# Expert up-products of a fused RWKV and two-stage MoE kernel: order of the first products, their waits, and the place of one row load

## The reference, cut to what matters

```python
for e in range(E):                       # 8 experts
    mask = e_idx == e                    # argmax of x @ w_gate
    h = np.maximum(x[mask] @ w1[e], 0.0) # 384 -> 1024
    ye = h @ w2[e]                       # 1024 -> 384
    out[mask] = gate_w[mask, None] * eom[mask, e, None] * ye
```

## Time and profile before

| | us |
|---|---|
| median of three runs | 867.23 |
| the profiled execution | 865.66 |
| its span, first to last instruction | 863.8 |
| TensorE busy | 842.6 (98%) |
| VectorE busy | 511.0 (59%) |
| ScalarE busy | 320.1 (37%) |

### The profile page before, as it was taken

The page is one execution under the profiler, slowest core; times in us unless marked ns, Lnnn a source line. Parts: engine busy times, 40 slices in busy tenths (PEclk is TensorE's granted clock), DMA queues, the critical chain, the costliest instruction groups (busy, mean ns, idle before and its releaser), DMA issues. The chain is left out here.

```text
span 863.8 us, 19737 instructions
## 1 busy us (share of the span) xinstructions
PE 842.6 (98%) x7827; PEld 728.3 (84%) x7827; DVE 511.0 (59%) x1123; ACT 320.1 (37%) x523; POOL 176.5 (20%) x139
## 2 busy tenths in 40 slices
PE   7999999999999999999999999999899999999995
PEld 5778888788777787778777878899899999999995
DVE  7868545444644354535443435369969777797770
ACT  4433231113111131113111221357457676686651
POOL 3333113311333033203220101003110111111010
PEclk9999999999999999999999999999999999999998
DMA  9443202211113012111200102447987668776700
GB/s 351 153 179 112 112 1 80 93 58 39 58 58 113 10 65 79 58 57 38 79 2 2 38 1 99 195 175 238 388 316 266 224 242 306 276 253 233 274 19 18
DMA packets 23714, 115.70 MB, mean 134 GB/s; under 512 B 3324, under 2 KB 9392, under 8 KB 18016
## 3 DMA queue, kind: packets, MB, share of 16 engines
q1 hardware_dynamic: 19552, 100.14, 32.0%
q0 software_dynamic: 3520, 9.87, 3.0%
q10 hardware_dynamic: 576, 4.72, 1.6%
HBM read 101.63 MB, written 14.16 MB: 134 GB/s over the span
## 5 line engine op out<-in xcount | busy, mean ns | idle before, releaser
L1225 DVE TENSOR_TENSOR PP<-SG,bank 128x512 f32<-128x512 f32 (+1 forms) x78 | 49.9, 646 | 211.3 <-issue 119.4
L1609 PE MATMUL bank<-X1H,WH 128*128 128x512 f32 x432 | 169.4, 393 | 2.2 <-DVE LG L1094 1.8
L1609 PE MATMUL bank<-X1H,WL 128*128 128x512 f32 x432 | 167.9, 390 | 0.0
L1609 PE MATMUL bank<-X1L,WH 128*128 128x512 f32 x432 | 167.9, 389 | 0.0
L774 ACT ACTIVATE SG<-bank 128x512 f32<-128x512 f32 x72 | 43.0, 598 | 243.8 <-PE bank L1609 243.8
L688 ACT ACTIVATE AH<-PP 128x512 fp32r<-128x512 f32 (+1 forms) x78 | 46.1, 598 | 162.6 <-DVE PP L1225 162.6
L1609 PEld LDWEIGHTS bank<-X1H,WH 128*128 128x128 f32 x432 | 81.0, 188 | 23.4 <-issue 7.1
L1609 PEld LDWEIGHTS bank<-X1H,WL 128*128 128x128 f32 x432 | 81.0, 188 | 17.3 <-DVE WL L1042 0.3
L1228 DVE TENSOR_TENSOR AL<-PP,AH 128x512 fp32r<-128x512 f32 (+1 forms) x78 | 65.2, 843 | 51.0 <-ACT AH L688 51.0
L1609 PEld LDWEIGHTS bank<-X1L,WH 128*128 128x128 f32 x432 | 81.1, 188 | 16.1
L1655 PE MATMUL bank<-AH,WH 128*128 128x512 f32 (+1 forms) x234 | 92.7, 396 | 0.0
(11 more groups left out here) (223 smaller groups left out, 1799.3 us busy)
## 6 DMA issues: line engine op xcount, KB each, us to landing
W_EVEN<-w SPq DMA_DIRECT2D x20, 1536.0 KB, 8.1
W_ODD<-w SPq DMA_DIRECT2D x18, 1536.0 KB, 7.5
RK_IN<-unit_rk SPq DMA_DIRECT2D x20, 736.0 KB, 4.3
V_IN<-unit_v SPq DMA_DIRECT2D x20, 448.0 KB, 3.4
STG<-w_dense ACTq DMA_DIRECT2D x4, 1152.0 KB, 5.5
XG_ODD<-store SPq DMA_DIRECT2D x9, 394.0 KB, 7.5
store<-PAD SPq DMA_DIRECT2D x8, 394.0 KB, 5.2
STG<-w_dense SPq DMA_DIRECT2D x2, 1152.0 KB, 8.3
```

The source lines that it names most:

```text
L1225: return tt(PP[:, part], SG[:, part], VALUE_PS[:, part], ALU.mult)
L1609: last = mm(bank_[:, :], lhs[:, f, m, k * P:k * P + P], rhs[:, k, :], start=(x == 0), stop=(x == len(terms) - 1))
```

## The change

On TensorE, the first block (f = 0) of a full tile is done in another order. For tile n = 2 (`weights_late`): wait for XH and all of W1H; three products WH by XH; wait for XL; three products WH by XL; then for each k a wait for that piece of W1L and the product WL by XH. For the other 11 full tiles: wait for XH and all of W1L; three WH by XH; three WL by XH; wait for XL; three WH by XL. Blocks f > 0 and half tiles keep their order. On SyncE, the rows of the first late tile are issued between its w1 and its w2, so the waits for the plan, the records and the pads now stand ahead of w2.

```diff
-            def load_weights(tile, e):
+            def load_w1_when_free(tile, e):
                 sp.wait_ge(w1_low, 3 * tile.n - 3)
                 sp.nop(nofuse=True)
                 load_w1(e, tile.buffer)
+
+            def load_w2_when_free(tile, e):
                 sp.wait_ge(w2_low, 2 * tile.n - 2)
                 sp.nop(nofuse=True)
                 load_w2(e, tile.buffer)
...
             sp.wait_ge(experts_ready, 1)
             sp.nop(nofuse=True)
-            load_weights(first, late_expert(0))
+            e = late_expert(0)
+            load_w1_when_free(first, e)
             sp.wait_ge(plan_ready, 1)
             sp.wait_ge(records_sent, 1 + CH)
             sp.wait_ge(pad_written, 16 * NE)
             sp.nop(nofuse=True)
             load_rows_when_free(first, late_row(0))
+            load_w2_when_free(first, e)
             load_tile(second, late_row(1), late_expert(1))
...
             def expert_up(tile, fs=range(ET)):
                 wh, wl = W1H[tile.buffer], W1L[tile.buffer]
+                weights_late = isinstance(tile.n, int) and tile.n == EARLY - 1
                 if fs[0] == 0:
-                    pe.wait_ge(w1_low, 3 * tile.n + 3)
-                    pe.wait_ge(x_low, tile.after)
+                    if tile.half_tile:
+                        pe.wait_ge(w1_low, 3 * tile.n + 3)
+                        pe.wait_ge(x_low, tile.after)
+                    else:
+                        pe.wait_ge(x_high, tile.after)
+                        pe.wait_ge(*((w1_high, 3 * tile.n + 3) if weights_late else (w1_low, 3 * tile.n + 3)))
...
+                    elif f > 0:
+                        for k in range(KT):
+                            mm(to, wh[:, w[k]], XH[:, k, :], start=(k == 0), stop=False)
+                            mm(to, wh[:, w[k]], XL[:, k, :], start=False, stop=False)
+                            last = mm(to, wl[:, w[k]], XH[:, k, :], start=False, stop=(k == KT - 1))
+                    else:
+                        for k in range(KT):
+                            mm(to, wh[:, w[k]], XH[:, k, :], start=(k == 0), stop=False)
+                        if weights_late:
+                            pe.wait_ge(x_low, tile.after)
+                            for k in range(KT):
+                                mm(to, wh[:, w[k]], XL[:, k, :], start=False, stop=False)
+                            for k in range(KT):
+                                pe.wait_ge(w1_low, 3 * tile.n + k + 1)
+                                last = mm(to, wl[:, w[k]], XH[:, k, :], start=False, stop=(k == KT - 1))
                         else:
+                            for k in range(KT):
+                                mm(to, wl[:, w[k]], XH[:, k, :], start=False, stop=False)
+                            pe.wait_ge(x_low, tile.after)
+                            for k in range(KT):
+                                last = mm(to, wh[:, w[k]], XL[:, k, :], start=False, stop=(k == KT - 1))
```

More of the change, by code:

```diff
@@ L527, in load_tile @@
             def load_tile(tile, row, e):
-                load_weights(tile, e)
+                load_w1_when_free(tile, e)
+                load_w2_when_free(tile, e)
                 load_rows_when_free(tile, row)
@@ L1680, in expert_up @@
                     to = H_PS[f // 2][:, (f % 2) * SLOT:(f % 2 + 1) * SLOT]
[L1681 to L1685, removed]
-                        else:
-                            mm(to, wh[:, w], XH[:, k, :], start=(k == 0), stop=False)
-                            mm(to, wh[:, w], XL[:, k, :], start=False, stop=False)
-                            last = mm(to, wl[:, w], XH[:, k, :], start=False, stop=(k == KT - 1))
+                    w = [slice(k * EF + f * P, k * EF + f * P + P) for k in range(KT)]
@@ new lines, in expert_up @@
+                    if tile.half_tile:
+                        for k in range(KT):
+                            mm(to, wh[:, w[k]], XS[:, k, :, :].rearrange("p a t -> p (a t)"), start=(k == 0), stop=False)
+                            last = mm(to[:, 0:HALF], wl[:, w[k]], XS[:, k, 0, :], start=False, stop=(k == KT - 1))
+                    elif f > 0:
[13 more added lines that the diff above has]
+                                last = mm(to, wl[:, w[k]], XH[:, k, :], start=False, stop=(k == KT - 1))
+                        else:
+                            for k in range(KT):
+                                mm(to, wl[:, w[k]], XH[:, k, :], start=False, stop=False)
+                            pe.wait_ge(x_low, tile.after)
+                            for k in range(KT):
+                                last = mm(to, wh[:, w[k]], XL[:, k, :], start=False, stop=(k == KT - 1))
```

## The result

The changed kernel takes 860.99 us, the median of four runs (860.57 to 861.18), and the kernel before 866.93 us on the same chip (four runs, 865.78 to 867.71). The ratio is 0.9931, with a 95% interval of 0.9919 to 0.9943: 0.69% faster, 5.9 us, where 2.6 us were forecast.

What follows compares the result with a forecast made beforehand. TensorE, busy 842.6 of 863.8 us, bounds the kernel, so only its holes can be won: 0.91 + 1.70 = 2.6 us off the median 867.23 gives 864.6 us, 0.30% faster; range 863.7 to 866.7 us.

Steps and rivals of the forecast that it cites:

- both holes that it priced: TensorE's waits at tile 2's first products (gain 0.91 us) and before turning tile 3's rows (gain 1.70 us).
- the request that does not move: SyncE still issues tile 3's rows at about 612.5; only w2 ahead of them in the DMA queue goes.
- its cover: Slack at ScalarE's copy of tile 3's w2: landing at about 620.1 instead of earlier was to cost nothing.
- The point from which it decides: Tile 3's w2 landing after 624.8 delays its down-products, one microsecond for each beyond; rival of a slower kernel, chance 0.03.
- the weight loads: Rival: the new order adds three loads in each of 12 tiles, 4.1 us, giving 868.7 us; chance 0.01.
- the midstream waits: Rival: waits inside the first blocks of twelve tiles cost 0.12 to 0.36 us each, 1.4 to 4.3 us; chance 0.06.
- In the other 11 full tiles the order changes but no wait goes.: First blocks outside tile 2: XL is ready at 623.29, products start at 627.78 in tile 3, so no gain.
- The head of the loop turn: TensorE starts 0.41 us apart there and not 0.17, read as the upper price of a midstream wait, 0.36 us with restart.
- TensorE's busy time has no holes: From 619.3 us on TensorE is busy 235.08 of 235.60 us, so nothing else of the changed code waits there.
- A loss of 1.70 us: Before turning tile 3's rows: the turning could start at 617.02 but starts at 618.72, the whole taken as gain.
- an offset of both kernels: The profiled execution lies 1.6 us below the median of the runs, so 863.1 us became 864.6 us.
- what SyncE waits for last is the plan: On SyncE ahead of the rows' request: a wait of 1.8 us for the plan (STI) gates it.

Runs made afterwards that it cites:

- f4: The changed kernel with w1 of the second late tile issued ahead of w2 of tile 3: 862.34 us, ratio 0.9945 to the kernel before.
- f3: The changed kernel with the wait for XL ahead of the first product again in the 11 full tiles, new order kept: 863.93 us, ratio 0.9964.
- e1: The changed kernel with the 11 full tiles other than tile 2 back in the old order and waits: 865.29 us, ratio 0.9951.
- f2: The changed kernel run once more without an edit: 860.6 us, ratio 0.9922 to the kernel before.
- E3: The kernel before with only the rows of tile 3 issued between its w1 and w2: 864.04 us, ratio 0.9926.

## Why the prediction was right and where it was wrong

**Right: both holes that it priced, for the execution that it priced them in.** 0.91 + 1.70 = 2.61 us were forecast and 2.65 measured; the order, the starts, the one fine wait that is still not met in time, the request that does not move, the turning at 616.75 (616.1 plus the 0.6 by which this execution runs later) are as forecast. The rows took 2.9 us and not 3.5, with no effect, since TensorE got there 0.7 us later than they did. W2 landed at 622.9 and not 620.1, 2.8 us later than forecast, because it took 9.3 us from its request and not 7.1; its cover took this up. The point from which it decides, 624.8, was about right: f4's w2 came 0.7 us after it and cost 0.94, where the prediction's rule of one for one gives 0.7. The lower bound of the range comes to 864.0 by its own terms (864.6 - 0.11 - 0.5) and not to 863.9; nothing hangs on it. Of the rivals, the weight loads did not grow, and the midstream waits cost nothing where they are met.

**The step that failed: "In the other 11 full tiles the order changes but no wait goes."** It rests on XL of tile 3, 4.5 us ahead of its products. But tile 3 follows a full tile. Seven of the 11 follow a half tile: a tile's rows are turned ahead of the previous tile's down-products, and behind a half tile these are 24 products, 4.27 us, and not 48, 8.43. VectorE has W1L's third piece, an index cast and XL to do in that time and ends 0.11 us too late (655.07 against 654.96), which with the 0.13 from there to the product is the hole of 0.24. The evidence was in the rows. The head of the loop turn was read as the price of a wait in midstream, an upper end of a cost, when it was a wait that the change could take away: 7 x 0.36 = 2.5 us. "TensorE's busy time has no holes" hid it: a product's row of 0.34 us covers 0.17 us of a 0.24 us hole, so that seven of them show as 0.5 us of idle time (235.60 - 235.08), which was read as nothing. What made it hard to see is that the waits' table put it down to "issue". In the trace the wait is met at 655.11 by an instruction of TensorE's sequencer that has no releaser in the table, and the product at 655.20 follows it. The Trainium skill, Perfetto Trace Analysis, "Sequencer-only Instruction (DRAIN, etc)", says that the profiler reports only the execution of such an instruction and not its wait; the trace agrees, as that instruction's row is only 0.04 us long and starts 0.04 us after the end of XL. In f3 the same wait is listed with 0.2 us and VectorE's name.

**Mis-sized: the rows' hole.** "A loss of 1.70 us" was right for one execution, which had the smallest of the four profiled holes at the old place (1.5, 2.4, 3.4, 5.3 us). The forecast took the distance of that execution to the median, 1.6 us, as an offset of both kernels. The changed kernel's profiled execution lies only 0.4 us below its median, so most of that distance was no such offset. The likely cause is this term, a longer hole and the clock behind it, which the changed kernel does not have; no trace of the timed executions shows it. The timed runs fit: ten of the changed kernel, in two sets, all lie between 860.3 and 861.2 us, while the medians of the kernel before go from 865.70 to 870.60. The reading "what SyncE waits for last is the plan" was also one execution's. B alone was worth 0.74% in its set, and 0.2% was forecast for it.

**Still open.** The pads' landing varies from execution to execution, and what delays it was not tried. The two full tiles of before whose products follow each other after 0.118 us and not 0.113 (8.59 and 8.56 us and not 8.28) have their like, one or two, at the heads of all six profiles with a hole of 0.24 us or more there, and at those of none of the other eight. Tile 2 does the same in e1, f2, f3 and f4 (8.78 us in the last three), and not in the changed kernel's own profile. Every such phase follows a hole at its start, at a granted clock of 1.00, but most phases behind such a hole do not do it; what makes them was not found. E3 (B alone) ran faster than e1 (A and B), by 0.25% of their ratios and 0.14% of their medians, though the traced spans differ by 0.2 us the other way. The two intervals overlap by a little, and two of e1's six runs lie at 867.17 and 868.43 while the other four lie between 864.85 and 865.44, so the difference may be none; it was not followed up.

## What to carry to other kernels

Check a claim "no wait goes" at each kind of neighbourhood, not at the first tile: here the slack behind a full tile was 4.5 us, and behind a half tile XL came 0.11 us too late. A gap of 0.2 us in TensorE's stream that repeats at the head of each turn and is put down to "issue" should be held against the end of what the head's waits name; one that ended 0.13 us after VectorE's last write was a wait here. Order a block's first products by what is ready and put each wait directly ahead of its first reader. And a hole whose releaser is a DMA is to be sized from several executions, with the clock behind it.

## What the runs showed of the hardware

The clock of TensorE stayed at 1.00 through holes up to 1.6 us and was granted at 0.5 behind those of 2.4, 3.4 and 5.3 us, at a further cost of 1.4 to 1.6 us, nearly the same for all three. A transfer of 394 KB landed 1.0 to 1.1 us behind the 1536 KB ahead of it in four executions in which those landed anywhere from 617.6 to 622.7, and 0.9 to 2.1 us behind a w1 in five others; in the four in which w1 was in at most 1.0 us after the rows' request, the rows took 2.9 to 3.0 us from that request. The same load of 1536 KB (w1 of tile 3) took from 7.0 to 11.7 us in different executions. A product that waits costs its wait and 0.12 us more, at the heads (0.24 + 0.12) as at the earlier trace rows.
